# Attention and two feed-forward blocks on one core: six token tiles instead of five, and the first tile's attention in float32 without split operands

## The chip, the cores and the metric

The kernel runs on one core of one Trainium2 chip. The metric is the time of one execution on the device in microseconds (us), the median of several runs. Instructions run on TensorE (PE; PEld is its weight loading), VectorE (DVE), ScalarE (ACT) and GpSimd (POOL); SyncE (SP) issues the DMAs.

## What is computed

```python
batch, n_heads, seq, head_dim = (4, 8, 576, 64)
scores = scale * np.matmul(q, k.transpose(0, 1, 3, 2))
thresh = np.max(scores, axis=-1, keepdims=True) - tau
scores = np.where(scores >= thresh, scores, -1000000000.0)
attn = softmax(scores)                  # with 1e-9 added to the sum
x = matmul(attn, v)                     # as 2304 tokens x 512
h = x @ w_in                            # 512 -> 2048
x = (h * np.tanh(softplus(h))) @ w_out  # 2048 -> 512
g = x @ w_gate                          # 512 -> 1536
return (g * sigmoid(g) * (x @ w_val)) @ w_out2    # 1536 -> 512
```

(`softmax`, `softplus` and `sigmoid` stand here for lines of the reference.) All inputs are float32.

## The kernel before

**Split products.** Nearly every product is made of fp32r matmuls on operands split in two: a high part (ScalarE writes it) and a low part, the remainder (VectorE or GpSimd writes it). A dense product is three matmuls for each 128x128 block of weights: high by high, high by low, low by high (`product`, lines 564 to 566). In the attention the two parts lie in the two halves of the 128 partitions, so a score block takes two matmuls (`k_hi` and `k_lo` against the stacked `q_sp`), and the product with v nine for a head.

**Tiles.** The 2304 tokens are cut into five tiles (`TILES`); a tile goes through both feed-forward blocks, 68 units (`UNITS`) of 4 weight blocks, so 68 x 4 x 3 = 816 matmuls, each as wide as the tile. Tokens of a tile may belong to one or two batches; `cut` makes pieces of them, here 384 | 192, 256 | 320, 192 | 384, 128 | 448 queries. A piece has 8 heads.

**Attention of a head.** For each chunk of 128 queries (64 left over of two neighbouring heads share one): `scores` on TensorE into one of two pairs of PSUM banks; `rowmax` on VectorE; `thresh` on GpSimd and `exp` on ScalarE; `mask` on VectorE, which multiplies and sums; `eps` on GpSimd, `recip` on VectorE, `norm` on GpSimd. `scores` of chunk C waits for `mask` of chunk C - 2. Then `tpose` (TensorE, by turns of keys), `p_high` and `p_low`, `values`, `head_shift` and `head_add` (which add the two halves), and for a pair of heads `x_high` and `x_low`.

**Weights.** Each unit's weights come in raw, 256 KB, are split (`w_high` on ScalarE, `w_low` by turns on VectorE and GpSimd) and written to `scratch`, 512 KB; later tiles load the split ones, 512 KB. Every unit is split in the first tile; half of them are stored there, the other half are loaded raw and split again in the second tile and stored then (`kept_at`). The ring holds 7 units (`W_RING`).

**Order.** A planner (`Plan`) sets the order of the steps on each engine from durations and lags written in the code. The attention of tile t is woven into the units of tile t - 1, paced so that it ends at `PACE` = 0.8 of them. The attention of the first tile (`alone`) has nothing to be woven into; it is called the head below, and ends with the first matmul of unit 0. Steps that use the exp table stay out of the stretch of the 16 mish units. In the head transposes take turns on four PSUM banks.

## Time and profile before

| what | value |
|---|---|
| median of 3 runs | 1177.75 us (1173.86 to 1334.2) |
| profiled execution, its own time | 1177.69 us |
| its span | 1175.9 us |
| busy, share of span | PE 96%, PEld 87%, DVE 51%, ACT 49%, POOL 51% |
| DMA | 231.85 MB, mean 197 GB/s |

The span is the part of the execution in which the program's instructions run; 1.8 us of the time lie around it. The busy shares are averages over a head with little matmul work and a long dense part. Times below are in us from the start of the span. A row of a window gives the stretch, its length, then for PE, PEld, DVE, ACT and POOL the busy us and, in brackets, the instructions, then the granted TensorE clock (1.00 is 2.4 GHz, 0.50 is 1.2), the DMA engines' mean busy share and their GB/s. A matmul's duration is its latency: neighbours overlap, so the pace of TensorE is read from the starts. The dense stages of the tiles begin at 104.3, 301.5, 530.1, 771.9 and 1007.3.

### The profile page before, as it was taken

What the parts mean: (1) busy time and instruction counts of PE and PEld (TensorE: products, weight loads), DVE (VectorE), ACT (ScalarE), POOL (GpSimd) and SP (SyncE); (2) the same over time, 40 slices, a digit from 0 to 9 for tenths busy, and PEclk for the clock granted to TensorE, in tenths of its full rate; (3) what the DMA queues carried; (4) which work ended last, traced back from release to release, by engine and by line L of the source; (5) the groups of instructions that cost most, each with busy time, mean ns of one, the idle gap of its engine ahead of it and who ended that gap; (6) DMA issues with size and microseconds to landing.
All of it is one profiled execution on the core that took longest, in us unless ns stands there. A gap on an engine that the chain in (4) does not pass through costs nothing.

```text
span 1175.9 us, 17588 instructions
## 1 busy us (share of the span) xinstructions
PE 1128.5 (96%) x6096; PEld 1020.5 (87%) x6096; DVE 597.6 (51%) x1187; ACT 571.3 (49%) x1062; POOL 596.0 (51%) x777
## 2 busy tenths in 40 slices
PE   4667999999999999999999999999999999999998
PEld 4557999999999999998888888888888888999998
DVE  7883289886128877720287676200865552000220
ACT  6664778785456666613565455124544431330220
POOL 7663888987466666734554466324534432230220
PEclk9886999999999999999999999999999999999999
DMA  7311867766887676776554467656544445777673
GB/s 224 107 52 57 286 210 233 236 222 220 282 270 242 197 237 215 241 261 202 193 173 157 157 214 235 204 198 196 174 149 157 136 155 186 220 216 219 217 217 124
DMA packets 89512, 231.85 MB, mean 197 GB/s; under 512 B 10064, under 2 KB 27984, under 8 KB 89424
## 3 DMA queue, kind: packets, MB, share of 16 engines
q1 hardware_dynamic: 89280, 230.73, 60.7%
q8 instruction: 49, 0.80, 0.3%
q14 instruction: 39, 0.32, 0.1%
q10 hardware_dynamic: 144, 0.00, 0.0%
HBM read 190.32 MB, written 40.37 MB: 196 GB/s over the span
## 4 chain that ended last, share of the span: by engine, by line
PE 90%; POOL 4%; DVE 3%; issue 1%; ACT 1%; DMA 0%; SPq 0%; ACTq 0%; DVEq 0%
PE ps_m L564 23%; PE ps_m L566 23%; PE ps_m L565 23%; PE ps_x L617 7%; PE ps_s L588 3%; PE ps_s L589 3%; PE ps_x L629 3%; PE ps_x L628 3%; POOL p_t L941 1%; PE ps_m L617 1%; POOL k_lo L919 1%; DVE p_t L820 1%; PE ps_x L630 1%; DVE q_sp L807 1%; DVE nmax L813 1%
## 5 line engine op out<-in xcount | busy, mean ns | idle before, releaser
L564 PE MATMUL ps_m<-x_hi,w_sp 128*128 128x512 f32 (+2 forms) x800 | 301.9, 377 | 3.5 <-POOL x_lo L947 3.4
L566 PE MATMUL ps_m<-x_hi,w_sp 128*128 128x512 f32 (+2 forms) x800 | 296.5, 371 | 0.0
L565 PE MATMUL ps_m<-x_lo,w_sp 128*128 128x512 f32 (+2 forms) x800 | 296.1, 370 | 0.0
L564 PE MATMUL ps_m<-g_hi,w_sp 128*128 128x448 f32 (+2 forms) x560 | 211.5, 378 | 0.0
L565 PE MATMUL ps_m<-g_lo,w_sp 128*128 128x448 f32 (+2 forms) x560 | 207.1, 370 | 0.0
L566 PE MATMUL ps_m<-g_hi,w_sp 128*128 128x448 f32 (+2 forms) x560 | 207.1, 370 | 0.0
L820 DVE SCALAR_TENSOR_TENSOR p_t<-ps_s,thr,p_t 128x576 f32<-128x576 f32 x144 | 116.0, 816 | 119.8 <-ACT p_t L723 109.0
L564 PEld LDWEIGHTS ps_m<-x_hi,w_sp 128*128 128x128 f32 x800 | 150.8, 189 | 20.0 <-issue 4.0
L566 PEld LDWEIGHTS ps_m<-x_hi,w_sp 128*128 128x128 f32 x800 | 150.8, 188 | 18.1
L565 PEld LDWEIGHTS ps_m<-x_lo,w_sp 128*128 128x128 f32 x800 | 151.0, 189 | 15.3
L958 POOL TENSOR_TENSOR g_lo<-g_raw,g_hi 128x448 fp32r<-128x448 f32 (+2 forms) x80 | 96.2, 1204 | 97.9 <-ACT g_hi L749 97.5
L723 ACT ACTIVATE p_t<-ps_s,nmax 128x576 f32<-128x576 f32 x144 | 105.0, 741 | 60.7 <-DVE nmax L813 58.9
L732 ACT ACTIVATE p_hi<-ps_x 128x384 fp32r<-128x384 f32 (+8 forms) x220 | 101.9, 478 | 66.9 <-PE ps_x L617 62.4
L813 DVE TENSOR_REDUCE nmax<-ps_s 128x1 f32<-128x576 f32 x144 | 107.0, 752 | 36.8 <-PE ps_s L589 35.4
L941 POOL TENSOR_SCALAR p_t<-p_t,rcp 128x576 f32<-128x576 f32 x144 | 112.2, 781 | 25.7 <-DVE rcp L826 23.6
L745 ACT ACTIVATE g_raw<-ps_m 128x448 f32<-128x448 f32 (+2 forms) x80 | 44.5, 556 | 162.8 <-PE ps_m L566 162.8
L963 POOL TENSOR_TENSOR g_lo<-g_raw,g_hi 128x448 fp32r<-128x448 f32 (+2 forms) x60 | 71.6, 1193 | 99.6 <-ACT g_hi L761 98.3
L617 PE MATMUL ps_x<-ident,p_t 128*128 128x128 f32 x740 | 112.4, 280 | 8.0 <-POOL p_t L941 6.5
L931 POOL TENSOR_SCALAR thr<-nmax,ntau 128x1 f32<-128x1 f32 x144 | 44.4, 309 | 145.8 <-DVE nmax L813 144.5
L566 PEld LDWEIGHTS ps_m<-g_hi,w_sp 128*128 128x128 f32 x560 | 105.1, 188 | 12.7
L588 PE MATMUL ps_s<-k_hi,q_sp 128*128 128x288 f32 x320 | 97.6, 322 | 17.9 <-DVE p_t L820 9.7
L564 PEld LDWEIGHTS ps_m<-g_hi,w_sp 128*128 128x128 f32 x560 | 105.2, 188 | 10.6
(69 smaller groups left out, 1764.7 us busy)
## 6 DMA issues: line engine op xcount, KB each, us to landing
w_sp<-scratch SPq DMA_DIRECT2D x238, 512.0 KB, 3.8
scratch<-w_sp SPq DMA_DIRECT2D x68, 512.0 KB, 4.1
w_raw<-weights SPq DMA_DIRECT2D x102, 256.0 KB, 4.0
k_raw<-kt SPq DMA_DIRECT2D x64, 288.0 KB, 3.2
v_raw<-v SPq DMA_DIRECT2D x64, 160.0 KB, 3.2
q_raw<-qt SPq DMA_DIRECT2D x16, 192.0 KB, 3.4
out_t<-o_sb SPq DMA_DIRECT2D x8, 256.0 KB, 3.8
out_t<-o_sb SPq DMA_DIRECT2D x8, 224.0 KB, 3.5
```

The source lines that it names most:

```text
L564: nc.tensor.matmul(ps, w_h, x_h, start=first, stop=False)
L565: nc.tensor.matmul(ps, w_h, x_l, start=False, stop=False)
L566: return nc.tensor.matmul(ps, w_l, x_h, start=False, stop=last)
L588: nc.tensor.matmul(to, q, k_hi[:, head, cols], start=b == 0, stop=False)
L617: last = nc.tensor.transpose(to[:, c, at:at + P], keys, ident)
L723: act.activation(halves(p_t[:, slot, :]), s_banks(C), ACT.Exp, bias=nmax[:, slot:slot + 1]).then_inc(e_ready, 1)
L732: act.activation(to, from_ps, ACT.Copy).then_inc(p_hi_ready, 1)
L813: dve.tensor_reduce(nmax[:, slot:slot + 1], s_banks(C), axis=AX.XY, op=ALU.max, negate=True).then_inc(max_ready, 1)
L820: dve.scalar_tensor_tensor(p, s_banks(C), thr[:, slot:slot + 1], p, ALU.is_ge, ALU.mult, accum_out=sums[:, slot:slot + 1]).then_inc(mask_d ...
L941: pool.tensor_scalar(p_t[:, slot, :], p_t[:, slot, :], rcp[:, slot:slot + 1], 1.0, ALU.mult, ALU.mult).then_inc(norm_done, 1)
L958: pool.tensor_tensor(g_lo[:, f, cols], g_raw[:, f, cols], g_hi[:, f, cols].bitcast(F32), ALU.subtract).then_inc(g_lo_ready, 1)
L963: pool.tensor_tensor(g_lo[:, f, cols], g_raw[:, f, cols], g_hi[:, f, cols].bitcast(F32), ALU.subtract).then_inc(s_lo_ready, 1)
```

## The change

There are six tiles, of 256, 320, 384, 448, 512 and 384 tokens; the pieces become 256 | 320 | 384 | 192, 256 | 320, 192 | 384. The heads of the first tile load q, k and v into four buffers each (`q_f`, `k_f`, `v_f`) and aren't split. A score chunk is two float32 matmuls: each takes 64 rows of the array (the two partition halves hold copies of q and k) and makes one half of the keys. The transposed probabilities are copied once (`p_copy`), and the values of two heads are ten float32 matmuls, five for each head, one head in each half of the array's columns (`values_two`); both heads land in one bank, from which ScalarE writes `x_hi` and VectorE `x_lo`. Transposes of the head take turns on three banks. Woven heads work as before, and the planner's costs change a little.

```diff
-TILES = (384, 448, 512, 512, 448)
+SLOTS = 4
+
+TILES = (256, 320, 384, 448, 512, 384)
...
 def x_place(k):
-    return k % 4 if k < ALONE_USES else k % X_BANKS
+    return k % 3 if k < ALONE_USES else k % X_BANKS
...
+SWITCH = 0.025
...
+def matmul_time(n):
+    return max(0.112, 0.008 + n / 2300)
...
-        mm = 3 * (0.231 if N == 512 else N / 2400 + 0.015)
+        mm = 3 * matmul_time(N)
...
+                if H < ALONE_HEADS:
+                    slot = H % SLOTS
+                    if i == 0:
+                        pe.wait_ge(q_f_ready, H + 1)
+                        pe.wait_ge(k_f_loaded[slot], 16 * (H // SLOTS + 1))
+                    for half in range(2):
+                        rows = slice(half * DH, (half + 1) * DH)
+                        last = nc.tensor.matmul(s_banks(C)[:, half, :], q_f[rows, slot, i * P:(i + 1) * P],
+                                                k_f[rows, slot, half * HALF:(half + 1) * HALF], start=True, stop=True)
+                    last.then_inc(s_filled, 1)
+                    return
...
+            def values_two(j):
+                if j:
+                    pe.wait_ge(x0_lo_ready, j)
+                for H in (2 * j, 2 * j + 1):
+                    pe.wait_ge(v_f_loaded[H % SLOTS], 32 * (H // SLOTS + 1))
+                pe.wait_ge(p_copied, TURN0[2 * j + 2])
+                for c in range(KC):
+                    for e in range(2):
+                        slot = (2 * j + e) % SLOTS
+                        last = nc.tensor.matmul(values_bank()[e * DH:(e + 1) * DH, :], v_f[:, slot, c, :], p_f[:, slot, c, :],
+                                                start=c == 0, stop=c == KC - 1)
+                last.then_inc(pair_done, 1)
...
+            def q_scaled(H):
                 if H == 0:
                     act.wait_ge(scale_ready, 2)
...
+                act.wait_ge(q_f_loaded[H % SLOTS], 16 * (H // SLOTS + 1))
+                q = q_f[:, H % SLOTS, :]
+                act.activation(q, q, ACT.Copy, scale=q_scale).then_inc(q_f_ready, 1)
...
+            def p_copy(H, i):
+                act.wait_ge(t_filled, TURN0[H] + i + 1)
+                if H >= SLOTS:
+                    act.wait_ge(pair_done, (H - SLOTS) // 2 + 1)
+                act.activation(p_part(H, i, p_f[:, H % SLOTS]), turned(H, i), ACT.Copy).then_inc(p_copied, 1)
+
+            def x_high(t, j):
+                act.wait_ge(pair_done, j + 1)
+                act.activation(x_hi[:, j, 0:TILES[t]], values_bank(), ACT.Copy).then_inc(x0_hi_ready, 1)
...
+            def x_low(t, j):
+                dve.wait_ge(x0_hi_ready, j + 1)
+                dve.tensor_tensor(x_lo[:, j, 0:TILES[t]], values_bank(), x_hi[:, j, 0:TILES[t]].bitcast(F32),
+                                  ALU.subtract).then_inc(x0_lo_ready, 1)
```

**TensorE in the head.** Before, around the values of head 0 (`v_sp` and `p_hi` are the split operands, L617 the transposes):

```order
L588 MATMUL ps_s<-k_hi,q_sp 128x288
L589 MATMUL ps_s<-k_lo,q_sp 128x288
L617 MATMUL ps_x<-ident,p_t 128x128 x3
L617 MATMUL ps_m<-ident,p_t 128x128 x6
L628 MATMUL ps_x<-p_hi,v_sp 128x384
L629 MATMUL ps_x<-p_lo,v_sp 128x384
L628 MATMUL ps_x<-p_hi,v_sp 128x384
```

After, the first rows of the head up to the values of the first pair (L654 the scores, L701 the transposes, L713 the values):

```order
L654 MATMUL ps_s<-k_f,q_f 128x288 x8
L701 MATMUL ps_x<-ident,p_t 128x128 x8
L654 MATMUL ps_s<-k_f,q_f 128x288 x2
L701 MATMUL ps_m<-ident,p_t 128x128 x2
L654 MATMUL ps_s<-k_f,q_f 128x288 x2
L701 MATMUL ps_x<-ident,p_t 128x128 x8
L701 MATMUL ps_m<-ident,p_t 128x128 x2
L654 MATMUL ps_s<-k_f,q_f 128x288 x2
L713 MATMUL ps_m<-p_f,v_f 64x256 x10
```

Scores of four chunks stand first, and the values of a pair stand once, behind the transposes of both heads, where each head had values of its own.

**VectorE in the head.** Before, between the sixth and seventh head (L836 are the low parts of the probabilities, L807 that of q, L847 the addition of the halves):

```order
L836 TENSOR_TENSOR p_lo_b<-ps_m,p_hi_b 128x384 x2
L836 TENSOR_TENSOR p_lo_b<-ps_x,p_hi_b 128x384 x2
L836 TENSOR_TENSOR p_hi_b<-ps_m,p_hi_b 64x384
L820 SCALAR_TENSOR_TENSOR p_t,sums<-ps_s,thr,p_t 128x576
L813 TENSOR_REDUCE nmax<-ps_s 128x1
L807 SCALAR_TENSOR_TENSOR q_sp<-q_raw,q_scale,q_sp 64x192
L826 RECIPROCAL rcp<-sums 128x1
L820 SCALAR_TENSOR_TENSOR p_t,sums<-ps_s,thr,p_t 128x576
L847 TENSOR_TENSOR x_raw<-ps_m,moved 64x384
```

After, from the third pair's `x_lo` (L977) to the end of the head; L941 is the mask, L934 the row maximum, L983 a low part of weights:

```order
L977 TENSOR_TENSOR x_lo<-ps_m,x_hi 128x256
L947 RECIPROCAL rcp<-sums 128x1
L934 TENSOR_REDUCE nmax<-ps_s 128x1 x2
L941 SCALAR_TENSOR_TENSOR p_t,sums<-ps_s,thr,p_t 128x576 x2
L947 RECIPROCAL rcp<-sums 128x1
L934 TENSOR_REDUCE nmax<-ps_s 128x1
L947 RECIPROCAL rcp<-sums 128x1
L941 SCALAR_TENSOR_TENSOR p_t,sums<-ps_s,thr,p_t 128x576
L947 RECIPROCAL rcp<-sums 128x1
L977 TENSOR_TENSOR x_lo<-ps_m,x_hi 128x256 x2
L983 TENSOR_TENSOR w_sp<-w_raw,w_sp 128x512
```

What stood between the masks is gone but for one subtraction for a pair of heads; the last two follow the last mask.

**ScalarE at the first dense units.** Before (L770 the high part of weights, L745 mish, L749 the high part of its result):

```order
L745 ACTIVATE g_raw<-ps_m 128x384
L770 ACTIVATE w_sp<-w_raw 128x512
L749 ACTIVATE g_hi<-g_raw 128x384
L708 ACTIVATE k_hi<-k_raw 128x576
L701 ACTIVATE q_sp<-q_raw,q_scale 128x192
L745 ACTIVATE g_raw<-ps_m 128x384
```

After:

```order
L860 ACTIVATE g_raw<-ps_m 128x256 x2
L885 ACTIVATE w_sp<-w_raw 128x512
L864 ACTIVATE g_hi<-g_raw 128x256 x2
L860 ACTIVATE g_raw<-ps_m 128x256
L885 ACTIVATE w_sp<-w_raw 128x512
L864 ACTIVATE g_hi<-g_raw 128x256
```

The three steps of a unit are the same; the mish and its high part are narrower, the weights' part as wide as it was.

## Rows read from the trace of the kernel before

**Rows 1.** Windows of the head and of the dense stages

```profile
core 0: us, PE busy (x) PEld busy (x) DVE busy (x) ACT busy (x) POOL busy (x), PEclk, DMA share, GB/s
11.20:90.40 79.20, 51.67 (x256) 45.18 (x256) 67.22 (x148) 51.42 (x93) 54.71 (x91) 0.88 0.39 122
104.30:301.50 197.20, 196.63 (x1248) 194.21 (x1249) 135.63 (x259) 136.98 (x266) 154.78 (x180) 0.99 0.70 228
301.50:530.06 228.56, 228.47 (x1322) 213.50 (x1321) 134.97 (x276) 130.69 (x254) 136.91 (x176) 1.00 0.73 240
530.06:1007.30 477.24, 477.24 (x2426) 406.79 (x2425) 229.68 (x454) 207.58 (x370) 208.72 (x288) 1.00 0.55 181
1007.30:1172.70 165.40, 165.40 (x817) 153.05 (x815) 19.98 (x32) 34.92 (x61) 32.32 (x28) 1.00 0.67 203
```

**Rows 2.** Groups of lines, VectorE alone, 11.2 to 90.4 us

```profile
L820 DVE SCALAR_TENSOR_TENSOR p_t<-ps_s,thr,p_t 128x576 f32<-128x576 f32 x24 | 19.2, 814 | 2.9 <-POOL thr L931 1.3 <-ACT p_t L723 1.0
L813 DVE TENSOR_REDUCE nmax<-ps_s 128x1 f32<-128x576 f32 x22 | 16.1, 753 | 1.5 <-PE ps_s L589 1.1
L807 DVE SCALAR_TENSOR_TENSOR q_sp<-q_raw,q_scale,q_sp 64x384 fp32r<-64x384 f32 (+1 forms) x8 | 6.1, 766 | 0.3
...
L826 DVE RECIPROCAL rcp<-sums 128x1 f32<-128x1 f32 x23 | 3.5, 157 | 1.3 <-POOL sums L936 0.8
L859 DVE TENSOR_TENSOR w_sp<-w_raw,w_sp 128x512 fp32r<-128x512 f32 x3 | 3.2, 1082 | 0.0
...
L820 DVE DVE_READ_ACCUMULATOR p_t<-ps_s,thr,p_t 128x1 f32 x24 | 2.0, 82 | 0.0
```

**Rows 3.** Timeline of the first scores: start, duration, engine, instruction

```profile
5.99 1.40 POOL L919 TENSOR_TENSOR k_lo<-k_raw,k_hi 128x576 fp32r<-128x576 f32 x1 [4.52 <-ACT k_hi L708]
...
7.90 0.58 PE L588 MATMUL ps_s<-k_hi,q_sp 128*128 128x288 f32 x1 [7.90 <-DVE q_sp L807]
...
11.22 0.82 DVE L820 SCALAR_TENSOR_TENSOR p_t<-ps_s,thr,p_t 128x576 f32<-128x576 f32 x1
```

**Rows 4.** Timeline at the end of the head

```profile
89.60 0.82 DVE L820 SCALAR_TENSOR_TENSOR p_t<-ps_s,thr,p_t 128x576 f32<-128x576 f32 x1 [0.81 <-ACT p_t L723]
...
98.17 0.52 PE L629 MATMUL ps_m<-p_lo_b,v_sp 128*128 128x384 f32 x1
...
98.49 0.52 PE L628 MATMUL ps_m<-p_hi_b,v_sp 128*128 128x384 f32 x1
...
104.32 0.66 PE L564 MATMUL ps_m<-x_hi,w_sp 128*128 128x384 f32 x1 [3.39 <-POOL x_lo L947]
```

**Rows 5.** Windows of one width of matmul, and the fullest ten microseconds of DMA

```profile
120.00:130.00 10.00, 10.00 (x59) 10.00 (x58) 3.29 (x3) 6.96 (x16) 9.37 (x8) 1.00 1.00 354
115.00:140.00 25.00, 25.00 (x146) 25.00 (x145) 6.24 (x6) 17.39 (x37) 22.89 (x20) 1.00 0.79 268
540.00:570.00 30.00, 30.00 (x134) 24.82 (x133) 0.00 (x0) 13.61 (x23) 14.23 (x11) 1.00 0.58 193
```

**Rows 6.** Timeline of TensorE: first and last start of runs of one width

```profile
108.85 0.29 PE L589 MATMUL ps_s<-k_lo,q_sp 128*128 128x288 f32 x1
...
109.38 0.29 PE L589 MATMUL ps_s<-k_lo,q_sp 128*128 128x288 f32 x1
...
229.83 0.28 PE L628 MATMUL ps_x<-p_hi,v_sp 128*128 128x256 f32 x1
...
230.54 0.28 PE L630 MATMUL ps_x<-p_hi,v_sp 128*128 128x256 f32 x1
...
363.09 0.30 PE L628 MATMUL ps_x<-p_hi,v_sp 128*128 128x320 f32 x1
...
363.96 0.31 PE L630 MATMUL ps_x<-p_hi,v_sp 128*128 128x320 f32 x1
```

**Rows 7.** Chain that ended last, a transpose group; start, time, what

```profile
265.16 0.66 PE ps_x L617 x6
```

**Rows 8.** Groups of lines by form, ScalarE, 104.3 to 301.5 us

```profile
L770 ACT ACTIVATE w_sp<-w_raw 128x512 fp32r<-128x512 f32 x64 | 40.2, 629 | 29.3 <-issue 15.2 <-PE ps_m L566 12.8 <-DMA w_raw<-weights 1.0
```

More of the change, by code:

```diff
@@ L212, in attention @@
                     pace = unit_end(UNITS * (tile - 1) + int(PACE * UNITS * (C - first) / (last - first)))
-                add("PE", 1.06 if e < 0 else 0.53, 1, ("scores", C), (("q_low", H), near), (("k_low", H), near),
-                    (("mask", C - 2), near), (pace, 0.0))
+                if alone:
+                    add("PE", 0.6, 0, ("scores", C), (("q_scaled", H), near), (("mask", C - 2), near))
+                else:
+                    add("PE", 1.06 if e < 0 else 0.53, 1, ("scores", C), (("q_low", H), near), (("k_low", H), near),
+                        (("mask", C - 2), near), (pace, 0.0))
                 add("DVE", 0.76, 5, ("rowmax", C), (("scores", C), 0.3))
                 add("POOL", 0.28, 0, ("thresh", C), (("rowmax", C), 0.1))
-                add("ACT", 0.74, 3, ("exp", C), (("rowmax", C), 0.1), (kept, 0.3), table="exp")
+                add("ACT", 0.74, 1 if alone else 3, ("exp", C), (("rowmax", C), 0.1), (kept, 0.3), table="exp")
                 add("DVE", 0.9, 2, ("mask", C), (("exp", C), 0.15), (("thresh", C), 0.1))
@@ L783, in _ @@
                     exp(*args)
+                elif step == "p_copy":
+                    p_copy(*args)
+                elif step == "x_high" and args[0] == 0:
+                    x_high(*args)
                 elif step == "p_high":
@@ L828, in p_low @@
             def p_low(H, i):
-                high, low = p_split(H)
-                dve.wait_ge(p_hi_ready, TURN0[H] + i + 1)
-                from_ps, hi = own(H, turned(H, i)), p_part(H, i, high)
+                dve.wait_ge(p_hi_ready, turns_before(H) + i + 1)
+                from_ps, hi = own(H, turned(H, i)), p_part(H, i, p_hi)
                 if i == len(turns_of(H)) - 1:
@@ L901, in _ @@
                     head_add(*args)
-                elif step == "x_high":
+                elif step == "x_low" and args[0] == 0:
+                    x_low(*args)
+                elif step == "x_high" and args[0]:
                     x_high(*args)
@@ L980, in _ @@
                     norm(*args)
-                elif step == "x_low":
+                elif step == "x_low" and args[0]:
                     x_low(*args)
```

198 lines of the change are left out of this document (127 added, 71 removed).

## The prediction

> **What bounds the kernel now.** I read the windows by stage first [rows 1]. In the four rows from 104.3 us on, TensorE is busy for all but 0.66 of 1068.4 us at the full granted clock, while no other engine passes 79% of a stage (GpSimd, 154.78 of 197.20). So that part is set by the number and width of the matmuls, and taking work from another engine there gives nothing. The head is different: between the first and the last mask TensorE is busy 51.7 of 79.2 us and VectorE 67.2, that is 85%. Nothing dense can start until the last head's x_low has been written; the first dense matmul starts at 104.32 [rows 4]. The time is therefore 104.3 (head) + 1068.4 (dense) + 3.2 (last copy and store) + 1.8 (around the span) = 1177.7 us, the profiled run's own time, equal to the median within 0.1. I price each part of the change in this sum.
>
> **The pace of TensorE by width.** Durations overlap, so I take starts. 288 columns: 0.53 us for four, 0.1325 each; 256 columns: 0.71 for six, 0.118; 320 columns: 0.87 for six, 0.145 [rows 6]. 384 and 512 columns: in a window two instructions straddle the ends, so 25 / 144 = 0.174 and 30 / 132 = 0.227 [rows 5]. 448 columns: 165.4 / 816 = 0.203 [rows 1]. A transpose: 0.66 / 6 = 0.11 [rows 7]; I take the same for a 128-wide matmul and 0.112 for 192, which must lie between 0.11 and 0.118.
>
> **Six tiles instead of five.** Each tile costs 816 matmuls. Before: 816 x (0.174 + 0.203 + 0.227 + 0.227 + 0.203) = 844 us. After: 816 x (0.118 + 0.145 + 0.174 + 0.203 + 0.227 + 0.174) = 849 or 850. The columns are the same 2304; what is added is the part of a matmul's pace that doesn't shrink with its width. Cost: **+6 us**, all on the path. It is this small because even 256 columns are still above the floor near 0.11.
>
> **More attention in the woven part.** Seven pieces are woven in both kernels, but with 2048 queries instead of 1920: pieces of 128 and 448 queries go, 320 and 384 come. Scores: 576 matmuls instead of 544, 32 x 0.1325 = 4.2. Transposes: 720 instead of 680, 40 x 0.11 = 4.4. Values: 72 x ((0.145 + 0.174) - (0.11 + 0.203)) = 0.4. Cost: **+9 us**. Check of the method on the kernel before: 844 + 72.1 (544 scores) + 74.8 (680 transposes) + 70.1 (504 value matmuls) = 1061, against 1068.4 measured, 7 or 8 us of waits and cold start. I keep 8 for the changed kernel.
>
> **The head: what VectorE keeps.** From the first to the last mask it had 24 chunks with low parts of p and q and additions between them. The changed order keeps 16 masks at 0.814 + 0.082, 14 row maxima at 0.753, 15 reciprocals at 0.157, three weight parts at 1.08, two q_low at up to 1.02 (the mean in the row is 0.766 over two widths), and two x_low of a pair, 128x256, which no row shows: between the 0.157 of one column and the 0.814 of 576, about 0.45 [rows 2]. Sum: 14.3 + 10.5 + 2.4 + 3.2 + 1.9 + 0.9 = 33.2 us. At the 85% of before this takes 39 us. The ring of score banks doesn't allow much more: scores, row maximum, exp and mask follow each other, and only then is the bank free again.
>
> **The head: start and end.** The first score waited for k_lo (5.99 + 1.40) and q_low and started at 7.90; the first mask came 3.3 us later [rows 3]. Without the low parts the first score can start when q is scaled and k is in, near 6.2, and the first mask come near 9. So the last mask ends near 9 + 39 = 48. Behind the last mask of before lie 104.3 - 90.4 = 13.9 us [rows 4], nine value matmuls for each of two heads at a pace of 0.32 for 384 columns (the 1.2 GHz level; 0.174 at 2.4) among them. After: eps, reciprocal and norm 1.3, transposes and three copies 2.5, values of the last pair 2.4 to 4.3, x_high and x_low 1.0. I take 8. The first dense matmul then starts near **56** (50 to 62), instead of 104.3: **-48 us**.
>
> **The price of float32 matmuls** is in no row: the only float32 instructions are transposes. Bounds for a chunk's scores: from two matmuls at the fp32r pace, side by side, 0.13, to eight one after the other when cold, 8 x 0.24 = 1.92. I take what a chunk costs now, four paces, 0.53 warm and 0.96 cold, since the work that the splits did must be done inside. For the values of a pair the same gives 5 x 4 x 0.118 = 2.4 warm and twice that cold, between ends of 0.6 and 9. TensorE has room for it, because it is idle or cold for much of the head (granted clock 0.88 there, [rows 1]); only the last pair's values lie bare on the path. "FP8 and Floating Point Precision" of the Trainium skill, TensorE Precision Notes, says that true float32 takes four passes through the array; by it the sum would be the same. No row here shows it.
>
> **Covers that get thinner.** In the first dense stage ScalarE still makes the high parts of some 62 units' weights at 0.629 [rows 8], 39 us, whatever the tile's width. With 20 exps, 40 copies of p, the high parts of q, k and v, and the dense steps at 256 columns I count about 115 us of work on it, against 97 + 12.7 + 13.2 + 10.4 = 133 us of matmuls; before it was 137.0 against 193. That is 86% where it was 71%; VectorE and GpSimd come to about 83%. While the 16 mish units run, a unit takes TensorE 12 x 0.118 = 1.42 us and ScalarE 0.629 + 0.39 + 0.41 = 1.43: no slack at all, and GpSimd and VectorE stand behind it in the same chain. Seven units of split weights stand ready, so not all of it is lost. I add **5 us** (0 to 14). In the second stage, DMA: 34 raw loads, 34 stores and 34 reloads of units and 8 heads are 50.3 MB in some 159 us, 316 GB/s, where the same stage ran at 240 before; the most that any ten microseconds show is 354 at a share of 1.00, without a loss on TensorE [rows 1, 5]. I add **2 us** (0 to 15).
>
> **The sum.** 56 + 1068.4 + 6 + 9 + 7 + 3.2 + 1.8 = **1151 us**, 2.3% under the 1177.7. By stage from the first dense matmul: 139, 160, 194, 229, 225, 142.
>
> **Rivals.**
> - *Crowding.* The first two stages are set by ScalarE and by DMA. If ScalarE can be driven no harder than the 78.5% that GpSimd reached [rows 1], stage one takes 115 / 0.785 = 146; if DMA holds 290 GB/s, stage two takes 173. Together 20 us more: 1171. For it: the counts above, and that three engines are near the limit together. Against it: 300 GB/s and more were carried without a wait, and a ring of seven units.
> - *The halves of the array don't run side by side.* Each pair of float32 matmuls in row or column halves then runs one after the other: a chunk's scores 1.1 to 1.9 us, a pair's values 4.7 to 9. About 1 us for each chunk, part hidden behind VectorE, and 4 at the end: head 73, time 1168. Nothing in the trace speaks on it.
> - *Slower than before.* The same, and the array cold through the whole head: 16 x 1.92 + 80 x 0.22 + 4 x 9 = 84 us of matmuls in one row with waits between them, so that the head, not VectorE, is set by TensorE and ends near 98: 1193 us, 1.3% slower. It is slower from a head of 83 us on. For it: the clock stood at 1.2 GHz at the end of the head of before. Against it: it would need both halves of the price at their upper end, and the array then has less idle time than now.
> - *Quicker.* The clock stays high, the masks follow closer and the crowding stays covered: head 50, no added waits, 1138.
>
> "TensorEngine Tiling (Array Packing)" of the Trainium skill, Key Properties, has a rule against this change: a change of tiling mode drains TensorE. The order of the head has 22 changes between row halves, whole array and column halves. A drain priced by the rows is a duration less a pace, 0.29 - 0.13 = 0.16 us, so 3.5 us in all, most of it in TensorE's idle time; it would fit in the range of the head.
>
> **How the numbers follow.** The forecast has 0.62 (its own range 1143 to 1160), crowding 0.12, no overlap of halves 0.13, quicker 0.10, slower than before 0.03. The range 1139 to 1170 leaves out the far ends of the rivals, some 2 in 10. 2% is about what a measurement of this kernel can tell from no change, and the border is 1154.2, close above the forecast: faster by more 0.54 (two thirds of the forecast's case, and the quicker one), within 2% 0.43, slower by more 0.03.
>
> **What would show it.** The first dense matmul between 50 and 62; first mask near 9 and last near 48, with VectorE busy about 85% between them; a chunk's two score matmuls starting together and lasting four paces; dense stages as above, the excess in the first two; 142 us in the last, pure 384-wide stage. The prediction is wrong if the head ends past 65, or if stages one and two together pass 310.

## The result, and the profile after

The changed kernel took 1167.23 us (median of 5 runs, 1165.34 to 1172.2), the kernel before beside it 1174.89 (5 runs); the ratio is 0.9939, with a 95% interval of 0.9921 to 0.9956. That is 0.6% faster, where 2.3% was forecast. One of the five runs of the kernel before (1334.2 us) fell in a slower state of the chip and is left out of the ratio. Two lines of the changed kernel's page, the busy times and the raw weight loads:

```profile
PE 1131.8 (97%) x6920; PEld 1059.3 (91%) x6920; DVE 583.1 (50%) x1192; ACT 568.7 (49%) x1112; POOL 578.5 (49%) x789
w_raw<-weights SPq DMA_DIRECT2D x102, 256.0 KB, 4.4
```

The windows by stage, which answer to [rows 1]:

```profile
8.00:51.90 43.90, 34.24 (x180) 20.79 (x181) 28.28 (x69) 28.27 (x55) 27.95 (x52) 0.88 0.70 225
51.90:61.10 9.20, 6.04 (x38) 3.95 (x37) 0.91 (x3) 3.15 (x8) 1.91 (x4) 0.81 0.31 93
61.10:204.50 143.40, 135.68 (x1083) 132.25 (x1084) 102.08 (x197) 100.54 (x212) 115.95 (x137) 1.00 0.80 274
204.50:379.90 175.40, 165.99 (x1127) 163.30 (x1126) 106.25 (x211) 99.35 (x196) 101.06 (x139) 0.97 0.83 284
379.90:573.00 193.10, 193.10 (x1251) 192.43 (x1250) 109.67 (x228) 102.96 (x202) 104.57 (x148) 1.00 0.73 240
573.00:801.10 228.10, 228.10 (x1321) 213.47 (x1320) 123.43 (x260) 112.64 (x222) 113.58 (x160) 1.00 0.63 205
801.10:1025.80 224.70, 224.70 (x1105) 190.57 (x1105) 91.98 (x186) 86.99 (x152) 84.21 (x116) 1.00 0.54 176
1025.80:1167.30 141.50, 141.50 (x817) 141.31 (x816) 17.90 (x32) 31.53 (x61) 28.32 (x28) 1.00 0.74 237
```

Four of the six dense stages are what the prediction has for them, and TensorE doesn't pause there: 193.1, 228.1, 224.7 and 141.5 us, against 194, 229, 225 and 142. The two first are not: 143.4 and 175.4 against 139 and 160. In the two together TensorE is idle for 17 us (7.7 and 9.4), and in part of the second it ran at a lower granted clock.

**The head** shrank from 104.3 to 61.1 us. This profiled run took 1172.2 us, 5 more than the median; two later kernels with the same order in the head (e3 and e4 below) began the first dense matmul at 56.6 and 56.8, three others (e5, e6 and e11, two of them with one GpSimd instruction more) at 57.8 to 58.6. With 56.7 the sum is 56.7 + 1106.2 (dense) + 3.1 (last copy and store) + 1.8 = 1167.8, the median. That the median run began there is an assumption, since only the run of 1172.2 us was profiled. What differs in the trace is TensorE's granted clock: e3's two windows of the head, to set beside the first two above, have 0.96 and 1.00 where those have 0.88 and 0.81.

```profile
8.00:48.40 40.40, 31.08 (x177) 18.52 (x177) 28.27 (x69) 27.94 (x54) 27.62 (x52) 0.96 0.69 217
48.40:56.60 8.20, 5.01 (x43) 3.80 (x41) 0.91 (x3) 3.49 (x8) 2.35 (x4) 1.00 0.35 106
```

The start of the head in the timeline, beside [rows 3] (the lines of 0.85 and 0.72 us are windows at one instant, which show what runs then), and the groups of its float32 matmuls:

```profile
5.03 2.29 PE L654 MATMUL ps_s<-k_f,q_f 64*128 64x288 f32 x8 [5.03 <-ACT q_f L800]
...
5.03 0.85 PE L654 MATMUL ps_s<-k_f,q_f 64*128 64x288 f32 x2 [5.03 <-ACT q_f L800]
...
5.64 0.72 PE L654 MATMUL ps_s<-k_f,q_f 64*128 64x288 f32 x2
...
6.12 0.72 PE L654 MATMUL ps_s<-k_f,q_f 64*128 64x288 f32 x2
...
6.60 0.72 PE L654 MATMUL ps_s<-k_f,q_f 64*128 64x288 f32 x2
...
8.03 0.81 DVE L941 SCALAR_TENSOR_TENSOR p_t<-ps_s,thr,p_t 128x576 f32<-128x576 f32 x1
...
22.77 1.97 PE L713 MATMUL ps_m<-p_f,v_f 128*64 128x256 f32 x8
...
L654 PE MATMUL ps_s<-k_f,q_f 64*128 64x288 f32 x64 | 15.9, 610 | 13.7 <-DVE p_t L941 8.6 <-ACT q_f L800 5.0
```

The 16 chunks have 32 score matmuls, and the group counts 64: a float32 matmul is recorded as two pieces. The eight pieces that begin at 5.03 are two whole chunks. They start in pairs, at 5.03, 5.64, 6.12 and 6.60, one piece of each half of the array within 0.04 us of the other: the halves run side by side. From pair to pair it is 0.48 us once they run, two paces of 0.24; so a matmul of two pieces takes four paces, and a chunk 0.96, the price for a cold array. The window from 0 to 8 us prints a granted clock of 1.00 all the same; the pace is that of the 1.2 GHz level. The values of a pair take 0.43 us from pair to pair of pieces at 22.77, twice 0.213, and 0.22 us at 49.15. What the engines wait for between the first and the last mask (engine, line, what was waited for: us in total, times, longest):

```profile
DVE p_t L941 <- ACT p_t L828: 11.2, 7, 4.1
...
ACT w_sp L885 <- DMA w_raw<-weights: 4.5, 2, 2.3
ACT k_hi L813 <- DMA k_raw<-kt: 3.1, 1, 3.1
```

VectorE is busy for 28.28 of 43.90 us and waits 11.2 for exp; ScalarE meanwhile stands, in its own order, ahead of loads of weights, q and k that haven't landed, with the exps queued behind. Three of the seven waits, 8.7 us together, follow such a stand directly; the longest, 4.1 us, one ahead of k.

**The boundary of the first two stages**, from the chain of waits (start, us, what):

```profile
209.56 0.61 PE ps_x L724
...
212.33 0.44 ACT moved L856
212.79 0.51 DVE x_raw L967
213.39 0.99 DVE x_hi L973
...
214.45 0.87 POOL x_lo L1074
215.36 0.63 PE ps_m L635
...
219.08 1.28 ACT L860
220.37 0.45 ACT g_raw L860
```

The tile of 320 tokens starts at 204.5, but the values of its last head are computed at 209.56, inside its own unit 0: in the planned order they stand there. Their sum, x_high (0.99 us) and x_low (0.87 us) follow with nothing for TensorE to do; then the table load and the first Mish (1.28 and 0.45 us, behind an exp) free the bank that the next unit waits for. The window shows what that leaves of TensorE, and its clock:

```profile
204.50:209.50 5.00, 3.10 (x23) 2.53 (x21) 2.35 (x6) 1.67 (x4) 0.95 (x2) 1.00 0.86 306
...
210.00:220.00 10.00, 6.93 (x28) 6.53 (x27) 3.66 (x6) 3.19 (x5) 2.33 (x3) 0.51 0.18 59
```

TensorE is idle for 1.9 us of the five before 209.5, still at a clock of 1.00; then come 28 matmuls in 10 us, at the 1.2 GHz level, with another 3.1 us idle among them.

### The profile page after: what moved, and what is told of

It reads as the page before. It is cut to its first block, busy times and chain, and to the rows that moved or that the text cites. A ratio compares the mean times of both kernels' runs of the same rounds, so it can differ in the third digit from the quotient of the medians.

```text
span 1170.4 us, 19484 instructions
## 1 busy us (share of the span) xinstructions
PE 1131.8 (97%) x6920; PEld 1059.3 (91%) x6920; DVE 583.1 (50%) x1192; ACT 568.7 (49%) x1112; POOL 578.5 (49%) x789
## 4 chain that ended last, share of the span: by engine, by line
PE 82%; POOL 6%; DMA 4%; DVE 3%; ACT 1%; issue 1%; SPq 1%; ACTq 0%; DVEq 0%
PE ps_m L635 21%; PE ps_m L637 21%; PE ps_m L636 21%; PE ps_x L701 6%; DMA w_raw<-weights 4%; PE ps_s L670 3%; PE ps_s L671 3%; PE ps_x L724 2%; PE ps_x L725 2%; POOL w_sp L1079 2%; POOL k_lo L1046 1%; POOL p_t L1068 1%; PE ps_m L713 1%; PE ps_x L726 1%; POOL g_lo L1085 1%
## 5 line engine op out<-in xcount | busy, mean ns | idle before, releaser
L635 PE MATMUL ps_m<-x_hi,w_sp 128*128 128x384 f32 (+4 forms) x960 | 330.0, 344 | 9.9 <-ACT g_raw L860 4.2
L637 PE MATMUL ps_m<-x_hi,w_sp 128*128 128x384 f32 (+4 forms) x960 | 323.3, 337 | 0.0
L636 PE MATMUL ps_m<-x_lo,w_sp 128*128 128x384 f32 (+4 forms) x960 | 323.0, 336 | 0.0
L635 PE MATMUL ps_m<-g_hi,w_sp 128*128 128x384 f32 (+4 forms) x672 | 230.6, 343 | 1.3 <-POOL g_lo L1085 0.8
L637 PE MATMUL ps_m<-g_hi,w_sp 128*128 128x384 f32 (+4 forms) x672 | 226.1, 336 | 0.0
L636 PE MATMUL ps_m<-g_lo,w_sp 128*128 128x384 f32 (+4 forms) x672 | 226.0, 336 | 0.0
L635 PEld LDWEIGHTS ps_m<-x_hi,w_sp 128*128 128x128 f32 x960 | 181.5, 189 | 19.7 <-issue 8.4
L637 PEld LDWEIGHTS ps_m<-x_hi,w_sp 128*128 128x128 f32 x960 | 181.3, 189 | 9.0
L941 DVE SCALAR_TENSOR_TENSOR p_t<-ps_s,thr,p_t 128x576 f32<-128x576 f32 x144 | 116.4, 816 | 145.0 <-ACT p_t L828 135.7
L1085 POOL TENSOR_TENSOR g_lo<-g_raw,g_hi 128x384 fp32r<-128x384 f32 (+4 forms) x96 | 100.0, 1047 | 99.3 <-ACT g_hi L864 99.3
L847 ACT ACTIVATE p_hi<-ps_x 128x384 fp32r<-128x384 f32 (+6 forms) x232 | 103.9, 464 | 70.3 <-PE ps_x L701 66.0
L635 PEld LDWEIGHTS ps_m<-g_hi,w_sp 128*128 128x128 f32 x672 | 126.6, 188 | 6.9 <-issue 1.6
L637 PEld LDWEIGHTS ps_m<-g_hi,w_sp 128*128 128x128 f32 x672 | 126.5, 188 | 6.5
L934 DVE TENSOR_REDUCE nmax<-ps_s 128x1 f32<-128x576 f32 x144 | 107.4, 752 | 48.9 <-PE ps_s L671 42.4
L636 PEld LDWEIGHTS ps_m<-g_lo,w_sp 128*128 128x128 f32 x672 | 126.7, 189 | 5.3
L860 ACT ACTIVATE g_raw<-ps_m 128x384 f32<-128x384 f32 (+4 forms) x96 | 46.9, 489 | 168.6 <-PE ps_m L637 168.3
L1090 POOL TENSOR_TENSOR g_lo<-g_raw,g_hi 128x384 fp32r<-128x384 f32 (+4 forms) x72 | 74.5, 1035 | 105.0 <-ACT g_hi L876 104.1
L701 PE MATMUL ps_x<-ident,p_t 128*128 128x128 f32 x784 | 119.0, 278 | 5.4 <-POOL p_t L1068 2.7
```

The costliest lines, as they stand in the source:

```text
L635: nc.tensor.matmul(ps, w_h, x_h, start=first, stop=False)
L636: nc.tensor.matmul(ps, w_h, x_l, start=False, stop=False)
L637: return nc.tensor.matmul(ps, w_l, x_h, start=False, stop=last)
L701: last = nc.tensor.transpose(to[:, c, at:at + P], keys, ident)
L847: act.activation(to, from_ps, ACT.Copy).then_inc(p_hi_ready, 1)
L860: act.activation(g_raw[:, f, 0:TILES[m]], m_bank(m, f), ACT.Mish).then_inc(mish_ready, 1)
```

## The experiments

Twelve kernels ran. The stages are read from the first dense matmul of each tile in the profiled run; "rest" is from the start of the third stage to the start of the last matmul. A median run can differ from the profiled one: the profiled runs of e1 and e3 were 3.0 and 2.8 us under their medians. Ratios are to the kernel before on the same chip.

| kernel | us | ratio, 95% | head | stage 1 | stage 2 | rest |
|---|---|---|---|---|---|---|
| before | 1174.9 | | 104.3 | 197.2 | 228.5 | 642.4 |
| changed | 1167.2 | 0.9939 (0.9921 to 0.9956) | 61.1 | 143.4 | 175.4 | 787.2 |
| e1 five tiles, new head | 1152.5 | 0.9792 (0.9769 to 0.9816) | 74.6 | 197.4 | 229.8 | 642.5 |
| e2 six tiles, old head | 1184.2 | 1.0065 (1.0044 to 1.0085) | 78.4 | 148.4 | 165.3 | 787.9 |
| e3 half the bytes | 1162.1 | 0.9875 (0.9851 to 0.99) | 56.6 | 139.9 | 170.5 | 787.2 |
| e4 pace 0.7 | 1168.1 | 0.9927 (0.9906 to 0.9948) | 56.8 | 145.0 | 173.9 | 787.5 |
| e5 thin low parts, half the bytes | 1152.8 | 0.9812 (0.9795 to 0.9829) | 57.8 | 133.3 | 168.7 | 787.2 |
| e6 tiles of 256 and 4 x 512 | 1194.1 | 1.0163 (1.0143 to 1.0183) | 57.8 | 202.6 | 252.7 | 674.2 |
| e7 tiles 384, 256, 320, ... | 1178.2 | 1.0023 (1.0009 to 1.0038) | 77.5 | 183.9 | 148.2 | 765.6 |
| e8 tiles 384, 3 x 512, 384 | 1149.2 | 0.9778 (0.9762 to 0.9794) | 75.0 | 204.0 | 249.3 | 614.3 |
| e9 six raw buffers | 1157.9 | 0.9857 (0.9836 to 0.9878) | 53.9 | 138.3 | 172.3 | 787.2 |
| e10 e8 with six raw buffers | 1150.2 | 0.9788 (0.9774 to 0.9803) | 77.1 | 204.0 | 249.4 | 614.3 |
| e11 thin low parts, all bytes | 1156.0 | 0.9836 (0.9821 to 0.9851) | 58.6 | 133.7 | 172.9 | 787.2 |
| e12 all low parts on VectorE | 1193.4 | 1.0152 (1.0124 to 1.0179) | 56.0 | 164.6 | 180.5 | 787.2 |

**e1 and e2: each half of the change alone.** e1 is the changed kernel, e2 the kernel before, with

```diff
-TILES = (256, 320, 384, 448, 512, 384)   # e1
+TILES = (384, 448, 512, 512, 448)
-TILES = (384, 448, 512, 512, 448)        # e2
+TILES = (256, 320, 384, 448, 512, 384)
```

Expected of e1: 

> The changed kernel with the five tiles of before (384, 448, 512, 512, 448): the float32 head alone. Both theories expect the dense stages of before, 1068 us from the first dense matmul to the last, since those stages had neither too many bytes nor too little room. The head of the changed kernel took 43.5 us between first and last mask for 16 chunks, 2.7 each, so 24 chunks give 65; with 8 in front and 10 behind it ends near 83. Time 83 + 1068 + 5 = 1156, ratio to before 0.984. If the float32 head itself spoils the first dense stage (its buffers lie in g_hi and g_lo), that stage is over 203 us instead of 197.

Expected of e2: 

> The kernel of before with the six tiles of the change and its split head. Theory DATA (stages one and two have nearly the bytes of before in less matmul time and wait for loads) and theory ORDER (the attention woven into stage one is late because the planner packs ScalarE, VectorE and GpSimd too tightly, and the second stage waits for it) both expect the dense part of the changed kernel, 1106 us, within 8. The split head for 16 chunks: 11 in front, 79.2 x 16/24 = 53 between the masks, 14 behind, 78. Time 78 + 1106 + 5 = 1189, ratio 1.012. If the new head's leftovers are the cause, the dense part is 1090 or less and the time under 1175.

The new head by itself brings 2.1%: it ends at 74.6 instead of 104.3 with all five dense stages as before, 8 us earlier than expected. The six tiles by themselves cost 0.65% in spite of a head of 78.4. So the two halves of the change have opposite signs, and what has to be explained is in stages one and two, the only ones that differ from the count of matmuls. The halves don't simply multiply: together they would give 0.9855, and 0.9939 was measured. The new head saves 30 us where it has 384 tokens to do (104.3 to 74.6) and 22 where it has 256 (78.4 to 56.7), and stages one and two are 5 us longer behind it than in e2.

e2 shows one thing more. Its order has the attention of the second tile complete before the boundary: its first stage holds 1104 matmuls, all that are due there, and the changed kernel's 1083. The twenty microseconds behind the boundary, in e2 and in the changed kernel:

```profile
226.80:246.80 20.00, 16.89 (x115) 16.40 (x114) 7.21 (x12) 11.95 (x25) 13.98 (x17) 1.00 0.84 277
```

```profile
204.50:224.50 20.00, 14.32 (x76) 13.15 (x75) 6.93 (x14) 8.01 (x16) 6.04 (x10) 0.74 0.47 160
```

TensorE still waits there (3.1 us idle in e2, 5.7 in the changed kernel), but the clock stays up, and stages one and two take 313.7 us together instead of 318.8. e2 differs in its head and the planner's costs too, so these 5 us are an indication and no measurement of the late attention alone.

**e3: half the bytes.** Only the high parts are stored and loaded again; the values are not the reference's.

```diff
-  sp.dma_start(scratch[G % UNITS], w_sp[:, G % W_RING, :, :].bitcast(F32))
+  sp.dma_start(scratch[G % UNITS, :, 0, :], w_sp[:, G % W_RING, 0, :].bitcast(F32))
...
-  sp.dma_start(w_sp[:, slot, :, :].bitcast(F32), scratch[u])
+  sp.dma_start(w_sp[:, slot, 0, :].bitcast(F32), scratch[u, :, 0, :])
```

> The changed kernel, but only the high part of a unit's split weights is stored and loaded again, so 256 KB each instead of 512; the low part that lies in the ring from an earlier unit is used in its place, so the values aren't the reference's. The order of all instructions is the same. DATA: the second stage falls from 175 to 160, the first from 143 to 138, time near 1150 (ratio 0.978). ORDER: nothing moves by more than 3 us, time 1164 to 1168.

The two stages fall by 3.5 and 4.9 us, 8.4 together, and the time, 1162.1 us, lies between what DATA and ORDER expected: neither is right alone. Bytes are a part of the loss and not the whole, and the pause at the boundary stays.

**e4: the pace.** `PACE = 0.8` became 0.7, so that the planner asks for the woven attention earlier.

> The changed kernel with PACE 0.7 instead of 0.8: the attention of the next tile is asked to end earlier. ORDER: the wait at the start of the second stage (TensorE had about 6 us of work in the 17 us from 204.5 on) goes, the second stage falls to 164, time near 1157. DATA: the attention is late because of loads, the crowding only comes earlier: first stage 3 to 6 longer, second 5 shorter, time 1163 to 1170.

Stages of 145.0 and 173.9 us, 318.9 instead of 318.8: nothing, so ORDER's 164 us for stage two is refuted, and so are DATA's shifts of 3 us and more. The 20 masks of stage one start 33.5 to 126.1 us behind its first matmul, in the changed kernel 33.9 to 125.4: the pace of 0.7 moved the attention by less than 1 us. (The time, 1168.1 us, is in DATA's range, and in that of no change.) The order keeps it behind the Mish units.

**e5 and e11: the splitting.** In both, the low parts of the weights are worked out for 8 of 512 columns, on VectorE and on GpSimd; e5 halves the bytes as e3 does, e11 doesn't.

```diff
-  w_sp[:, G % W_RING, 1, :], w_raw[:, r % W_RAW, :], w_sp[:, G % W_RING, 0, :].bitcast(F32),
+  w_sp[:, G % W_RING, 1, 0:8], w_raw[:, r % W_RAW, 0:8], w_sp[:, G % W_RING, 0, 0:8].bitcast(F32),
...
+  pool.memset(w_sp[:, :, 1, :].bitcast(F32), 0.0)
```

Expected of e5: 

> The changed kernel with its order, in which the low parts of the weights are worked out for 8 of 512 columns (the rest is set to zero once, at the start) and only the high parts are stored and loaded again; its values are not the reference's. It takes about 55 us from VectorE and 90 us from GpSimd in the first two stages beside the halved bytes, which alone gave 1162.1 us with stages one and two at 139.9 and 170.5 us. Theory B (crowding on the engines): stages one and two fall to 133 to 136 and 157 to 162 us, 1145 to 1152. Theory A (the order that was planned keeps the last head's transposes and values behind the boundary, and the chain behind them is waited for whatever else is idle): stages one and two stay at 137 to 140 and 166 to 170 us, the pause of about 10 us at the boundary is still there, 1157 to 1162.

Expected of e11: 

> The changed kernel with its order, in which the low parts of the weights are worked out for 8 of 512 columns (the rest is set to zero once, at the start), but stored and loaded again in full; its values are not the reference's. With half the bytes as well it took 1152.8 us, stages one and two 133.3 and 168.7 us; with half the bytes alone 139.9 and 170.5; the changed kernel 143.4 and 175.4. If bytes and splitting cost each for itself, stages one and two are 137 and 173 to 174 us, 1159 to 1161. If the bytes hurt only because the split that follows is late (one chain from the landing over ScalarE and the low part to TensorE, whose slack either of them gives back), this alone gives most of both: 134 to 135 and 169 to 171, 1153 to 1156.

The windows of stages one and two, first of e5, then of e11:

```profile
57.80:191.10 133.30, 132.44 (x1084) 131.70 (x1085) 74.62 (x197) 100.31 (x212) 71.20 (x138) 1.00 0.75 230
191.10:359.80 168.70, 163.25 (x1128) 161.83 (x1127) 95.38 (x210) 100.17 (x196) 81.50 (x138) 0.99 0.59 188
```

```profile
58.60:192.30 133.70, 132.54 (x1083) 131.74 (x1084) 73.45 (x195) 98.76 (x209) 70.72 (x136) 1.00 0.84 290
192.30:365.20 172.90, 165.18 (x1128) 162.42 (x1127) 95.22 (x212) 101.12 (x200) 81.92 (x139) 0.98 0.86 290
```

With bytes and order untouched, stage one falls from 143.4 to 133.7 us, and TensorE is busy for all but 1.2 of them, at 290 GB/s and with ScalarE as busy as before. So in stage one the splitting on VectorE and GpSimd was the loss, the bytes hardly: they bring 3.5 us while the low parts are there and 0.4 without them. That is the second answer in the expectation of e11, one chain whose slack either gives back. Stage two, 172.9 us, went by the first. In stage two it is the other way: 2.5 us for the splitting, 4.9 for the bytes, 6.7 for both, each for itself. And with both gone 168.7 us are left of stage two, with the pause in it: the chain of waits of e5 has at its boundary

```profile
197.71 0.44 ACT moved L856
198.17 0.51 DVE x_raw L967
198.77 0.99 DVE x_hi L973
199.83 0.87 POOL x_lo L1074
200.74 0.41 PE ps_m L635
```

the same five steps in the same 3 us. This third part is set by the order. In e5 each theory had one stage right: 133.3 us is B's first stage and 168.7 A's second, and the time lies between the two ranges.

**e6, e7 and e8: other widths**, in the changed kernel: (256, 512, 512, 512, 512), (384, 256, 320, 448, 512, 384) and (384, 512, 512, 512, 384).

Expected of e6: 

> The changed kernel with five tiles of 256 and four times 512 tokens: one tile less, and the head with 256 tokens kept. By the paces: head 57, stages 155, 244, 244, 244 and 185 us, 1131 in all with the end. Theory A (room): behind the Mish units the first stage has some 133 us for 32 chunks that take 4.5 to 5.4 us each, 144 to 172 us, so it and the boundary lose 15 to 40 us: 1148 to 1170. Theory B (crowding by weights): stage one is 22 us longer than in the changed kernel and stage two 70 us, so the loss is mostly gone: 1135 to 1142. Theory C (only the count of tiles costs): 1131 to 1137.

Expected of e7: 

> The changed kernel with the same six widths in another order: 384, 256, 320, 448, 512 and 384. As many dense matmuls as now and 128 fewer woven queries. By the paces of the trace (0.118, 0.146, 0.173, 0.200 and 0.227 us for 256, 320, 384, 448 and 512 columns, 816 of them a stage, and 1.83 us of woven work for 16 queries) the stages are 170, 133, 170, 228, 225 and 142 us behind a head of 75. Theory A (a stage of 256 tokens is too short for the next tile's attention, which then ends behind the boundary): stage one is wide here and its woven attention short, so it loses under 4 us, but the 256-wide second stage must still hold 320 queries and loses 8 to 12 us: 1153 to 1160. Theory B (weights crowd the transfers and the engines in the first two stages): those two together are a little shorter here than in the changed kernel in spite of the bytes being the same, so they lose as much as there, 25 us in both: 1166 to 1172. Theory C (only the count of tiles costs, by its 6 us): 1146 to 1149.

Expected of e8: 

> The changed kernel with five tiles of 384, 512, 512, 512 and 384 tokens. Against the five tiles of 384, 448, 512, 512 and 448 (1152.5 us) the dense matmuls take 4 us less by their paces and the woven queries are as many. Theory A (room for the attention): the first stage must now weave 512 queries in place of 448; at 4.5 to 4.9 us for a chunk its 32 chunks take 144 to 157 us, and the stage has some 166 us behind its Mish units, so it just fits: 1148 to 1151. Theory B (crowding by weights): stage one is longer, so a little better too, 1147 to 1149. If the first stage is short of room all the same, it shows transposes and values behind the boundary and 1155 to 1160.

Their first stages, and of e7 the second too, one window of each kernel in the order e6, e7, e8:

```profile
57.80:260.40 202.60, 175.35 (x1293) 165.69 (x1293) 145.05 (x286) 133.33 (x279) 150.90 (x189) 0.93 0.68 224
```

```profile
77.50:261.30 183.80, 183.80 (x1176) 183.05 (x1177) 109.08 (x211) 119.64 (x254) 134.63 (x144) 1.00 0.73 236
261.30:409.50 148.20, 138.38 (x1107) 136.20 (x1106) 87.12 (x188) 86.83 (x186) 88.96 (x123) 0.99 0.95 333
```

```profile
75.00:278.90 203.90, 202.24 (x1299) 200.24 (x1300) 144.67 (x285) 140.02 (x280) 158.06 (x189) 1.00 0.69 219
```

e6 is the clearest: 512 queries woven into a stage of 256 tokens leave TensorE idle for 27 us of it, with a granted clock of 0.93, 47 us over the sum of paces. One tile less bought nothing; 32 chunks don't fit into a stage of 256 tokens, and the values of its last two heads lie behind the boundary. This is theory A's direction, past the top of its range.

e7 fell outside every range, by my own sum. Its second tile takes the tokens 384 to 639, across the end of a batch at 576, so it has two pieces and sixteen heads; the window shows 1176 matmuls, 360 of them woven, and TensorE without any pause. Stage one was longer by work, 14 us, and lost nothing. Stage two, 256 tokens wide, took 148.2 us against 133: it lost 15, with DMA at a share of 0.95. So the loss goes with the narrow tile wherever it stands among the first two, and the sum of 25 that theory B expected isn't there. But theory A's cause isn't there either: the last values stand 2 us before the boundary, all 1104 matmuls lie in the stage (1107 in the window), and TensorE has no idle time behind it. What the trace shows inside the stage is

```profile
ACT w_sp L885 <- DMA w_raw<-weights: 34.8, 20, 4.0
```

that is, ScalarE stands 34.8 us ahead of raw weights, against 20.2 in the first stage of the changed kernel. So this loss of 15 us comes without any late attention; by these waits it is one of loads and splitting, which no run of this order with fewer bytes or shorter low parts confirms.

e8 has the lowest median of the study, 2.2% under the kernel before. Its interval overlaps those of e1 (0.9792) and e10 (0.9788). Its values of the last head lie 7 us behind the first boundary, the sign for which 1155 to 1160 us was expected; it took 1149.2.

**e9 and e10: six buffers for raw weights** (`W_RAW = 4` became 6) in the changed kernel and in e8, with the orders that the planner makes of it.

Expected of e9: 

> The changed kernel with six buffers for raw weights in place of four, and the order that the planner makes with them. Its order now has the values of the last two heads of tile one behind the boundary, in place of one. Theory L (in stages one and two TensorE waits because raw weights land late, 4.4 us in the median and up to 8.75): two more buffers take about half of the 8 us that the bytes cost, and stages one and two, 143.4 and 175.4 us, sum to 312 to 315: 1161 to 1164 us. Theory E (the engines that split the weights, and the chain of the late attention, are what is waited for, and earlier loads only move the crowding): the sum stays at 317 to 323, 1166 to 1172 us.

Expected of e10: 

> Five tiles of 384, 512, 512, 512 and 384 tokens (1149.2 us) with six buffers for raw weights in place of four. Its first two stages took 204.0 and 249.3 us with losses of 7 us each, of which 3 are there in every stage with woven attention. Theory L: 2 to 4 us of the rest go, 1145 to 1147. Theory E: 1148 to 1151.

e9 takes stage one from 143.4 to 138.3 and stage two from 175.4 to 172.3, 310.6 together, a little better than theory L had it, and its median is 9 us lower; about a third of that is a shorter head, the order of which also changed (in the profiled run 53.9 us, with the granted clock at 1.00 throughout). e10 changes nothing, 204.0 and 249.4 us. By these two runs raw buffers are short where a stage is 256 tokens wide and not where it is 384.

**e12: all low parts on VectorE.**

```diff
 def low_on_vector(r):
-    return r % 2 == 1
+    return True
```

> The changed kernel with the low part of every weight group worked out on VectorE, in place of every second one on GpSimd, and the order that the planner makes with it; its order has the last two heads of tile one behind the boundary. In the changed kernel 6 of VectorE's 51 low parts ran while no GpSimd operation did and took 0.69 us, and 18 that ran wholly beside long GpSimd operations took 1.24 us in the mean. Theory P (VectorE and GpSimd hold each other up when both read and write SBUF, and that is what makes the splitting dear): all low parts take 0.7 to 0.8 us, VectorE's busy time in stage one rises by under 20 us, GpSimd's falls by 41 us, and stages one and two, 143.4 and 175.4 us, come to 136 to 140 and 171 to 174: 1155 to 1162 us. Theory V (VectorE is what is short, and its busy time alone counts): with 15 to 20 us more of it the first stage takes 146 to 155 us and the boundary more, 1170 to 1185 us.

Both theories gave too little: 1193.4 us, stage one 164.6. The group of low parts in stage one, with what VectorE waited for ahead of them, in the changed kernel and then in e12, and e12's first stage whole and in three stretches:

```profile
L983 DVE TENSOR_TENSOR w_sp<-w_raw,w_sp 128x512 fp32r<-128x512 f32 x32 | 31.4, 980 | 22.2 <-ACT w_sp L885 21.9
```

```profile
L983 DVE TENSOR_TENSOR w_sp<-w_raw,w_sp 128x512 fp32r<-128x512 f32 x64 | 44.9, 714 | 36.8 <-ACT w_sp L885 36.5
...
56.00:220.60 164.60, 142.71 (x1065) 136.61 (x1065) 114.39 (x226) 100.16 (x207) 74.70 (x105) 0.94 0.74 248
...
56.00:104.00 48.00, 47.91 (x396) 47.71 (x397) 22.27 (x34) 29.57 (x65) 15.60 (x18) 1.00 0.86 284
104.00:160.00 56.00, 48.15 (x366) 46.89 (x365) 40.66 (x84) 35.42 (x72) 23.86 (x30) 0.94 0.81 272
160.00:220.60 60.60, 46.65 (x309) 42.01 (x307) 51.46 (x110) 35.17 (x70) 35.25 (x58) 0.89 0.59 197
```

Theory P was right on the durations, 714 ns in place of 980, and on GpSimd, 41 us less; twice as many low parts cost VectorE only 12 us of busy time. The stage is longer all the same, with VectorE busy for 114.4 of 164.6 us, no larger share than before. One thing that grew is the time that VectorE stands still in its order, ahead of a low part whose high part isn't there: 36.5 us instead of 21.9. Busy and standing still together are 124 of 143.4 us in the changed kernel, 86%, and 151 of 164.6 in e12, 92%.

But the order is another one too, and that can't be told apart here. In e12 the first mask of the woven attention starts 59.1 us into the stage, behind 410 dense matmuls, where it was 33.9 us and 246. Up to 104 us TensorE loses 0.1 us; the idle time of 22 us lies wholly behind, where the 20 chunks have 105 us left, and the values of the last two heads end behind the boundary. So e12 shows that GpSimd's relief shortens a low part, and that this kernel with its new order is slower; it doesn't show that VectorE's standing is what makes it slower.

## Why the prediction missed

**What bounds the kernel; the paces; six tiles; more attention.** Right. The four stages behind the second are within 1 us of their forecasts, and the head and dense stages still add up to the time.

**The head.** The step "start and end" was right: 56.6 us in e3 where 56 was said, first mask at 8.0 (said 9), last mask ended at 48.4 there (said 48); the tail took 8.2 (said 8). The profiled run of the changed kernel itself was some 4.5 us longer in the head, at a lower granted clock. The step "what VectorE keeps" was wrong in two ways that cancel: it keeps less than 33.2 us (28.28 busy in the window) at a share of 64%, not 85% (70% in e3, 28.27 of 40.40). The list of instructions and their durations was right, 32.6 us counted in the same way; but records overlap, so that the busy time is less than their sum, and I divided the one by a share that was made of the other. The engine that is waited for is ScalarE, which stands ahead of loads. I carried over a share that belonged to a VectorE full of low parts.

**The price of float32.** Right: four paces, and the halves of the array side by side; that rival (0.13) is refuted by the trace. The rule of the Trainium skill that true float32 takes four passes ("FP8 and Floating Point Precision", TensorE Precision Notes) agrees with the trace, four paces of 0.24 us for 288 columns. "TensorEngine Tiling (Array Packing)" of the Trainium skill states under Key Properties that a change of tiling mode drains TensorE; no run here measured that alone. Heads of 53.9 to 58.6 us with such changes in them (22 in the changed kernel) leave no room for a large price, but the 3.5 us that I put on it would fit.

**Covers that get thinner: the step that failed.** It added 5 and 2 us; without it my sum has 292 us for stages one and two, measured were 318.8. So the two covers were worth 27 us, four times what I took and close to the sum of the upper ends, 29. The term was seen and mis-sized, and its reason was half right:
- *Splitting and its loads, 10 us in stage one* (143.4 to 133.7 in e11). I put this on ScalarE and counted 115 us of work for it; it was busy 100.54, 70%, and stayed at 98.76 when the loss had gone. Nor was it lost where I saw no slack, at the Mish units: of the 7.7 us that TensorE was idle in the changed kernel's stage one, 1.1 lie in the first 24.9 us, 4.9 in the next 62.0 and 1.8 in the last 56.5.

```profile
61.10:86.00 24.90, 23.81 (x193) 23.48 (x194) 8.76 (x9) 18.17 (x42) 18.41 (x20) 1.00 0.65 211
86.00:148.00 62.00, 57.14 (x452) 55.13 (x451) 48.76 (x97) 44.53 (x90) 51.58 (x65) 1.00 0.81 278
148.00:204.50 56.50, 54.73 (x442) 53.65 (x441) 44.56 (x93) 37.84 (x81) 45.96 (x54) 1.00 0.85 298
```

My reading is that the loss is in the round of a raw buffer: landing, high part, low part on VectorE or GpSimd behind other work, and only then the next load. In the changed kernel's first stage ScalarE waited 20.2 us in 14 pieces for raw weights; in the first stage of before all but 1.0 us of its waits ahead of the same step were for TensorE or for nothing that the profile shows. Smaller transfers (e3), more buffers (e9) and shorter low parts (e11) each give some of the loss back, and with it the wait falls, to 14.1, 18.1 and 12.7 us; in the narrow second stage of e7 it is 34.8. That they act through this one round is argued from these waits; each effect is measured.
- *Bytes in stage two, 5 us* (e3), against the 2 that I took; stage two moved 284 GB/s on the average.
- *The attention that ends late, 7 to 10 us.* This wasn't in the prediction at all. With bytes and splitting out of the way (e5) the two stages still take 302 us, 10 over the 292, and the chain of waits shows the pause. I had priced the woven attention by its matmuls and never asked if its chain fits. In the changed kernel's stage one the first mask starts 34 us in, behind the Mish units, the last of 20 at 125 us, 4.8 us from one to the next, and the values of the last head at 151: the stage has 143.

```profile
L941 DVE SCALAR_TENSOR_TENSOR p_t<-ps_s,thr,p_t x20: 805/815/819, 95.0 to 186.5; 128x576 f32<-128x576 f32 x20
```

In e6, with 32 chunks, the last mask starts at 179 us, and the stage is 47 us over its sum. How much is gained when it does fit isn't measured: e2, where it does, is 5 us quicker in the two stages and still 21 over the 292.

**The rivals.** The one called crowding, with a chance of 0.12, said 146 and 173 us for the two stages, 319 together, and 1171; measured were 318.8 and 1167.2. The size was there, and what I set against it holds at 290 GB/s, which e11 carried through its first stage with TensorE idle for 1.2 us; at 333 GB/s, in the second stage of e7, TensorE was idle for 9.8. What it had wrong is the engine. Its low chance was the mistake: three engines at 80% and more, by my own count, in chains that wait for each other in order are a reason for its price, not for a small addition (measured in stage one: ScalarE 70%, VectorE 71%, GpSimd 81%). The mark that I set for being wrong, stages one and two past 310, was passed, the other, a head past 65, wasn't. One sum of the chances is off as well: two thirds of 0.62 and the 0.10 of the quicker case make 0.51, not 0.54.

**Where the gain went.** With the start that e3 and e4 have, the head gave 47.6 us, as forecast; the dense part took back 38 of them, 1106.2 against 1068.4, where I had 22. Of these 38, 15 are the added matmuls and queries. With five tiles (e1) nearly nothing is taken back, and the head still ends at 74.6.

**Open:** how the pause at the boundary would be removed. A pace of 0.7 didn't do it. e2 has an order with the attention complete before the boundary, and a shorter wait there; the changed kernel was never run with such an order. Nor was an experiment made on the drain between tiling modes.

## To carry to other kernels

A narrower first tile shortens a head that nothing covers, but the work that doesn't shrink with the width (splitting each weight once, a chain of steps for each chunk, a load's landing) then has less time to hide in; compare for each stage its length with that work's full round, waits in order included, and not only with busy times. When an engine has 70% of busy time, look at what it stands still for in its order before calling it free. And measure the two halves of a change apart where they can be: here one was worth 2.1% and the other cost 0.65%, and five tiles of 384, 512, 512, 512 and 384 tokens (e8, 2.2% under before) had the lowest median, with e1, five tiles of 384 to 512, within its interval.
